# Attention, expert mixture and gated layer on one core: the last expert and last layer take one token pair at a time

## What is computed

```python
# experts: x (2304, 512), w1 (8, 512, 1024), w2 (8, 1024, 512), P (2304, 8) balanced over 8 rounds
out = sum(P[:, e:e+1] * (np.maximum(x @ w1[e], 0.0) @ w2[e]) for e in range(8))
# last layer: w_gate, w_val (512, 1536), w_out (1536, 512)
xn = out / np.sqrt(np.mean(out * out, axis=-1, keepdims=True) + 1e-6) * rms_g
g = xn @ w_gate
y = (g / (1 + np.exp(-g)) * (xn @ w_val)) @ w_out
```

## Time and profile before

| | us |
|---|---|
| median of 3 runs | 2183.65 |
| lowest, highest | 2183.62, 2208.83 |
| profiled execution, device time | 2198.95 |
| its span, first to last instruction | 2197.2 |
| mean granted TensorE clock, share of full | 0.987 |

### The profile page before, as it was taken

The page is one execution under the profiler, slowest core; times in us unless marked ns, Lnnn a source line. Parts: engine busy times, 40 slices in busy tenths (PEclk is TensorE's granted clock), DMA queues, the critical chain, the costliest instruction groups (busy, mean ns, idle before and its releaser), DMA issues.

```text
span 2197.2 us, 28136 instructions
## 1 busy us (share of the span) xinstructions
PE 2117.6 (96%) x10780; PEld 1890.1 (86%) x10780; DVE 1357.6 (62%) x2452; ACT 750.4 (34%) x1816; POOL 338.6 (15%) x362
## 2 busy tenths in 40 slices
PE   8987999999999999999999999999999689999998
PEld 6777989789898989989898989899988578888887
DVE  3676576555656565656565556556556766666666
ACT  3663222423233323233223233232234533333332
POOL 3351010000000000000000000000001433333332
PEclk9999999999999999999999999999999889999999
DMA  4320001000000100000100000100000000000002
GB/s 128 115 85 1 20 20 34 20 20 25 20 20 20 34 20 25 20 20 20 34 20 25 20 20 20 34 24 21 20 20 15 15 15 29 15 30 15 27 18 87
DMA packets 34517, 65.28 MB, mean 30 GB/s; under 512 B 3952, under 2 KB 5968, under 8 KB 34384
## 3 DMA queue, kind: packets, MB, share of 16 engines
q1 hardware_dynamic: 34384, 63.48, 8.9%
HBM read 58.75 MB, written 4.72 MB: 29 GB/s over the span
## 4 chain that ended last, share of the span: by engine, by line
PE 89%; DVE 4%; POOL 3%; ACT 3%; issue 1%; DMA 0%; SPq 0%; DVEq 0%; POOLq 0%; ACTq 0%
PE ps L1014 27%; PE ps L1015 27%; PE ps L1013 27%; PE ps L966 3%; PE ps L980 2%; POOL wa_raw L440 2%; POOL x_raw L417 1%; PE ps L992 1%; DVE x_lo L705 1%; DVE wa_lo L716 1%; PE ps L962 1%; DVE acc L780 1%; ACT x_hi L503 1%; ACT acc L561 1%; DVE h_sum L788 0%
## 5 line engine op out<-in xcount | busy, mean ns | idle before, releaser
L1013 PE MATMUL ps<-x_hi,wa_hi 128*128 128x384 f32 x1848 | 627.6, 340 | 58.5 <-DVE x_lo L705 27.9
L1014 PE MATMUL ps<-x_lo,wa_hi 128*128 128x384 f32 x1848 | 626.3, 339 | 0.0
L1015 PE MATMUL ps<-x_hi,wa_lo 128*128 128x384 f32 x1848 | 624.3, 338 | 0.0
L1015 PE MATMUL ps<-w_hi,h_lo 128*128 128x512 f32 x1368 | 542.5, 397 | 0.0
L1014 PE MATMUL ps<-w_lo,h_hi 128*128 128x512 f32 x1368 | 540.7, 395 | 0.0
L1013 PE MATMUL ps<-w_hi,h_hi 128*128 128x512 f32 x1368 | 534.2, 391 | 3.7 <-DVE w_lo L721 2.7
L773 DVE SCALAR_TENSOR_TENSOR acc<-ps,plan,acc 128x512 f32<-128x512 f32 x504 | 377.1, 748 | 139.8 <-PE ps L1015 139.5
L1013 PEld LDWEIGHTS ps<-x_hi,wa_hi 128*128 128x128 f32 x1848 | 350.3, 190 | 97.3 <-ACT h_sum L528 30.7
L1014 PEld LDWEIGHTS ps<-x_lo,wa_hi 128*128 128x128 f32 x1848 | 350.1, 189 | 28.1
L528 ACT ACTIVATE h_sum<-ps 128x384 f32<-128x384 f32 x396 | 193.3, 488 | 487.8 <-PE ps L1015 487.8
L1015 PEld LDWEIGHTS ps<-x_hi,wa_lo 128*128 128x128 f32 x1848 | 350.1, 189 | 0.0
(11 more groups left out here) (104 smaller groups left out, 1450.8 us busy)
## 6 DMA issues: line engine op xcount, KB each, us to landing
raw<-stream SPq DMA_DIRECT2D x164, 256.0 KB, 2.9
out<-acc SPq DMA_DIRECT2D x18, 256.0 KB, 2.1
v_sb<-v_loc SPq DMA_DIRECT2D x8, 384.0 KB, 4.2
q_sb<-q_str SPq DMA_DIRECT2D x8, 315.0 KB
k_sb<-k_str SPq DMA_DIRECT2D x8, 315.0 KB
v_sb<-v_str SPq DMA_DIRECT2D x8, 315.0 KB
k_sb<-k_loc SPq DMA_DIRECT2D x8, 304.0 KB, 3.4
q_sb<-q_loc SPq DMA_DIRECT2D x8, 288.0 KB, 2.8
```

The lines of the kernel that those rows point to most:

```text
L1013: nc.tensor.matmul(out_ap, a_hi, b_hi, start=first, stop=False, **free)
L1014: nc.tensor.matmul(out_ap, a_hi, b_lo, start=False, stop=False, **free)
L1015: return nc.tensor.matmul(out_ap, a_lo, b_hi, start=False, stop=last, **free)
```

## The change

From unit 28 on, the last expert, the order of steps is turned: all four units for pair 0, then for pair 1, then for pair 2 (steps 84 to 95); the same in the last layer, twelve units for each pair (steps 96 to 131). So every one of these 48 steps needs a new unit, and each is loaded and converted anew: 76 *fetches* instead of 44 units. In the last layer the w1 parts alternate between two buffers (`wa`, `wb`), the w2 chunk has four slots instead of three, the z bank and the gate and value tiles (`gv`, `sh_hi`, `sh_lo`) are doubled or fourfold.

x for the last layer is made over 7 to 9 steps for each pair (squares in steps 89, 97 and 108, norms and transposes in the two steps after, sums, high and low parts up to steps 95, 105 and 116).

In the last layer the outputs of two consecutive steps are accumulated in PSUM and added to `acc` once: three outputs of 6 matmuls in a step, at places 0, 2 and 4; none in step 97. Steps 130 and 131 have theirs singly. The output rows of a pair are stored when the pair is done.

The diff, cut to its core:

```diff
+UNITS_LAST = FC // 2
+FETCH_CYCLE = UNITS_MOE - UNITS_LAST
+FETCH_MOE = FETCH_CYCLE + TP * UNITS_LAST
+FETCHES = FETCH_MOE + TP * KC
+CYCLE = TP * FETCH_CYCLE
...
+def unit_of(s):
+    if s < CYCLE:
+        return s // TP
+    return FETCH_CYCLE + (s - CYCLE) % UNITS_LAST if s < MOE else UNITS_MOE + (s - MOE) % KC
...
 def w2_step(g):
-    u = unit_of_w2(g)
-    if u == 0:
+    f = fetch_of_w2(g)
+    if f == 0:
         return None
-    if u >= UNITS_MOE:
-        return TP * u - 1
-    return TP * u - 2 if g % 2 == 0 else TP * u + 1
+    if f >= FETCH_MOE:
+        return first_step(f)
+    if g % 2:
+        return first_step(f) + 1
+    return TP * f - 2 if f <= FETCH_CYCLE else first_step(f)
...
+SQUARES = [CYCLE + 5, MOE + 1, MOE + KC]
+SUMS = {0: {SQUARES[0] + 3: (0, 4)}, 1: {SQUARES[1] + 3: (0, 2), SQUARES[1] + 4: (2, 4)},
+        2: {SQUARES[2] + 3: (0, 2), SQUARES[2] + 4: (2, 4)}}
+SPLITS = {0: {SQUARES[0] + 4: (0, 3), SQUARES[0] + 5: (3, 5), SQUARES[0] + 6: (5, 7)}}
+for n_pair in (1, 2):
+    SPLITS[n_pair] = {SQUARES[n_pair] + 5 + i: (2 * i, min(2 * i + 2, 7)) for i in range(4)}
...
     GpSimd, step s (q = s - MOE)
         for s in range(STEPS):
+            f, q = fetch_of(s), s - MOE
+            if q >= 0:
+                if q:
+                    h_low(q - 1, 1)
+                    h_low(q - 1, 0)
                 pool.wait_ge(sig_done, 2 * q + 1)
+                nc.gpsimd.tensor_tensor(gv[:, q % 2, SIG0, :], gv[:, q % 2, GATE0, :], gv[:, q % 2, SIG0, :],
                                         ALU.mult).then_inc(silu0_done, 1)
+            if s == last_step(f) and f + 1 < FETCHES:
                 for k in range(4):
+                    w1_sum(f + 1, k)
...
     ScalarE, a last-layer step
+        def last_layer_step(s):
+            f, q = fetch_of(s), s - MOE
+            fetch = f + 1 < FETCHES
+            snap(s, 0)
+            if q:
+                h_high(q - 1, 0)
...
+            if fetch:
+                w1_high(f + 1, 0)
+                w1_high(f + 1, 1)
+            sigmoid(q, 0)
+            if fetch:
+                w1_high(f + 1, 2)
+                w1_high(f + 1, 3)
+            snap(s, 1)
+            more_x(s, 0)
+            if fetch:
+                w1_high(f + 1, 4)
+                w1_high(f + 1, 5)
+            snap(s, 2)
+            more_x(s, 1)
+            if fetch:
+                w1_high(f + 1, 6)
...
+            sigmoid(q, 1)
+            more_x(s, 2)
+            h_high(q, 1)
+            more_x(s, 3)
...
     VectorE, a last-layer step
+            if q:
+                product_0(q - 1)
...
+            early_x(s)
+            add(s, 0)
+            if fetch:
+                w1_low(f + 1, 0)
+                w1_low(f + 1, 1)
+            evac(s, 0)
+            if fetch:
+                w1_low(f + 1, 2)
+                w1_low(f + 1, 3)
+            evac(s, 1)
+            if fetch:
+                w1_low(f + 1, 4)
+                w1_low(f + 1, 5)
+            more_x(s, 0)
+            add(s, 1)
+            evac(s, 2)
+            if fetch:
+                w1_low(f + 1, 6)
...
+            evac(s, 3)
+            more_x(s, 1)
+            product_1(q)
+            evac(s, 4)
+            evac(s, 5)
```

More of the change, by code:

```diff
@@ L53 @@
 UNITS_MOE = E * FC // 2
[L54 to L79 removed]
+GROUPS = 2 * SUB
+ORDER = [3, 4, 5, 0, 1, 2]
@@ new lines, in outputs_of, with last_output @@
+def outputs_of(s):
+    return max(n for n, (steps, tok) in enumerate(OUTPUTS) if s in steps) + 1
+def last_output(tok, end):
+    return max(n for n, (steps, t) in enumerate(OUTPUTS) if t == tok and steps[-1] < end)
+SQUARES = [CYCLE + 5, MOE + 1, MOE + KC]
+SUMS = {0: {SQUARES[0] + 3: (0, 4)}, 1: {SQUARES[1] + 3: (0, 2), SQUARES[1] + 4: (2, 4)},
+        2: {SQUARES[2] + 3: (0, 2), SQUARES[2] + 4: (2, 4)}}
+SPLITS = {0: {SQUARES[0] + 4: (0, 3), SQUARES[0] + 5: (3, 5), SQUARES[0] + 6: (5, 7)}}
@@ new lines, in more_x @@
+        def more_x(s, k):
+            for p in range(TP):
+                if s == SQUARES[p]:
+                    for i in ((0, 1), (2,), (3, 4), (5,))[k]:
+                        square(p, i)
+                if s - SQUARES[p] in (1, 2):
+                    xt(p, DC * (s - SQUARES[p] - 1) + k)
+                first, end = SPLITS[p].get(s, (0, 0))
+                if first + k < end:
+                    x_high(TP + p, first + k)
+        for s in range(STEPS):
+            if s < MOE:
+                moe_step(s)
+            else:
+                last_layer_step(s)
@@ L659, in _ @@
+        h_high(TP * KC - 1, 0)
     @block.vector
@@ L936, in _ @@
-            if s:
-                evac(s, 5)
-            if fetch:
-                w1_low(u + 1, 6)
-            if before in range(TP):
-                mean_square(before, 0)
-            if now in range(TP):
-                for o in range(NPROD):
-                    x_low(TP + now, o)
+            low(s, 2)
+            if fetch:
+                w1_low(f + 1, 4)
+                w1_low(f + 1, 5)
+            evac(s, 4)
+            add(s, 2)
+            low(s, 3)
+            evac(s, 5)
@@ new lines, in last_layer_step @@
+        def last_layer_step(s):
+            f, q = fetch_of(s), s - MOE
+            fetch = f + 1 < FETCHES
+            if q:
+                product_0(q - 1)
+            else:
+                for g in range(W2_CHUNKS):
+                    if w2_step(g) == s and w2_late(g):
+                        w2_low(g)
+            early_x(s)
+            add(s, 0)
+            if fetch:
+                w1_low(f + 1, 0)
+                w1_low(f + 1, 1)
+            evac(s, 0)
+            if fetch:
+                w1_low(f + 1, 2)
+                w1_low(f + 1, 3)
+            evac(s, 1)
+            if fetch:
+                w1_low(f + 1, 4)
+                w1_low(f + 1, 5)
+            more_x(s, 0)
+            add(s, 1)
+            evac(s, 2)
+            if fetch:
+                w1_low(f + 1, 6)
+            for g in range(W2_CHUNKS):
+                if w2_step(g) == s and not w2_late(g):
+                    w2_low(g)
+            evac(s, 3)
+            more_x(s, 1)
+            product_1(q)
+            evac(s, 4)
+            evac(s, 5)
@@ new lines, in more_x @@
+        def more_x(s, k):
+            for p in range(TP):
+                if s == SQUARES[p] and k == 1:
+                    mean_square(p, 0)
+                first, end = SPLITS[p].get(s, (0, 0))
+                for o in range(first, min(first + 1, end)) if k == 0 else range(first + 1, end):
+                    x_low(TP + p, o)
+        for s in range(STEPS):
+            if s < MOE:
+                moe_step(s)
+            else:
+                last_layer_step(s)
+        product_0(TP * KC - 1)
@@ L946, in _ @@
+        for k in range(GROUPS):
+            evac(STEPS, k)
     @block.tensor
@@ L1162, in _ @@
             product(s, O_A22, y_up, False)
-            if s:
-                outputs(s, 5)
+            outputs(s, 5)
             between(s, 5)
+        for k in range(GROUPS):
+            outputs(STEPS, k)
     ctx.close()
```

535 lines of the change are left out of this document (277 added, 258 removed).

## The result

The changed kernel takes 2284.9 us (median of four runs, 2275.85 to 2304.55); the kernel before took 2190.71 beside it (2183.62 to 2208.83). The ratio is 1.043, with an interval of 1.032 to 1.054: slower. The profiled execution took 2275.85, its span is 2274.1, and the mean clock is 0.979 against 0.987.

What follows compares the result with a forecast made beforehand. Took TensorE's matmuls as the bound, with the change adding a wait to every last-layer step. 618 + 79 (wait) + 46 (smaller terms) + 20 (clock) = 763 against 682.7, +80, so 2264 us; range 2215 to 2310.

Steps and rivals of the forecast that it cites:

- The wait put into every last-layer step: Before S1, TensorE waits for ScalarE's copy behind w1 parts needing GpSimd's late sums: 33 steps x 2.4, 79 us.
- The clock: TensorE drops to 1.2 GHz after some waits: 12 to 13 falls, 20 us, bounds 0 to 55.
- TensorE's work alone, 618: From step 84 to the last matmul, matmuls and transposes without any waiting take 618 us, against 682.7 before.
- Norms: In steps 98, 99, 109 and 110 they precede VectorE's first add; the chain starts 2.0 later: 8 us.
- parts of x: Low parts in steps 102 to 104 and 113 to 115 make VectorE's next first add late: 10 us.
- step 96: Late w2 part, w1 load, table load and sigmoid chain put S1 at 13.3 instead of 7.0: 6.4 us.
- step 97: No output stands before S1, so the same chain makes the step 13.4 instead of 7.4: 6 us.
- end: After the last steps, the last product stands behind two evacuations: 1.8 us.
- GpSimd's sums of x: Two of 1.9 after the w1 sums end before GpSimd's next input comes, so they cost nothing.
- The w2 term: In the last expert, the second chunk's low part reaches output 0 late: 0.95 x 11 steps, 10.5 us.
- the blocking rule: Two-input VectorE and GpSimd instructions block each other in SBUF; low parts could each lose up to 0.7 more.
- Rival 1: The order does no harm: third GpSimd sum done by 5.0, S1 does not wait, -45, 2139 us; chance 0.10.

Runs made afterwards that it cites:

- experiment 1: Changed kernel with GpSimd's four w1 sums ahead of the second low part and the sigmoid's product in last-layer steps: 2202.3 us, ratio 1.003 to the kernel before.
- experiment 2: Changed kernel with ScalarE's copy for S1 ahead of w1 high parts 2 and 3 in last-layer steps: 2230.6 us (once).
- experiment 3: Changed kernel with one unused 128x384 GpSimd product ahead of the sigmoid's product in last-layer steps: 2330.3 us (once).
- experiment 4: Changed kernel with one unused 128x384 GpSimd product behind the four w1 sums in last-layer steps: 2278.6 us (once).
- experiment 6: Changed kernel with the second w2 chunk's high and low parts made one step earlier in the last expert and step 96: 2258.1 us (once).
- experiment 11: Changed kernel with w1 sums first, add before norm, w2 chunk early, last product before last evacuations, pair 0's x sums early: 2177.2 us, ratio 0.991 to kernel before.
- experiment 7: Changed kernel with GpSimd's w1 sums first, VectorE's first add ahead of the norm and the second w2 chunk early: 2167.4 us, ratio 0.989 to the kernel before.
- experiment 5: Changed kernel with VectorE's first add ahead of the norm's operations in last-layer steps: 2269.3 us (once).
- experiment 10: Changed kernel with GpSimd's sums of x for pair 0 (step 92) ahead of that step's w1 sums: 2302.1 us (once).

## Why the prediction was right

The forecast was 2264 us in a range of 2215 to 2310; the median is 2284.9. The profiled execution, the fastest of the four, is 12 above the forecast, which is the 12 by which the stretch came out longer (775.2 for 763). The other 9, up to the median, can't be placed, since the other executions have no profile; the start of step 84 alone differs by up to 26 between profiled ones. The mechanism is the one forecast; here is the sum against the measurement, with the clock taken out of the steps.

| us | forecast | measured |
|---|---|---|
| steps 84 to 95 | 203.5 | 211.5 |
| steps 96, 97 | 35.4 | 34.1 |
| steps 98 to 130 | 482.2 | 478.8 |
| step 131 and end | 21.6 | 21.7 |
| clock, all steps | 20 | 29.2 |
| sum | 763 | 775 |

**The wait put into every last-layer step: right.** Forecast 2.2 idle and a step of 13.9 from the durations of the earlier trace rows; measured 2.20 and 13.94. Two small errors inside the chain cancel: GpSimd's product takes 1.26 and not 1.02, and the sigmoid before it ends 0.11 earlier. The forecast also had 33 of them, and there are 33. The table of experiments 1 to 4 shows its cause, the sums behind the sigmoid and the copy behind the sums: take away either link and it goes or shrinks, lengthen it and it grows by the same amount, put the load elsewhere and nothing happens.

**The clock: right for the last layer, too low in all, and in part luck.** The forecast had 12 to 13 falls and 20 us, chosen between its bounds of 0 and 55 on the strength of two waits. In steps 98 to 130, 13 steps contain seven or more matmuls of 384 columns 0.32 apart (or of 512 columns 0.43 apart) instead of 0.175 (0.23); the excess over these spacings adds up to 21.6 us. Steps 93, 94, 96 and 97 have falls too, for another 3.7 and 3.9. Steps 122 and 127, 15.5 long with the same wait of 2.20 as their neighbours of 13.94, show one fall alone, 1.56 each. TensorE of the changed kernel in step 122, at the end of such a fall:
```profile
2132.28 0.52 PE L1231 MATMUL ps<-x_hi,wa_lo 128*128 128x384 f32 x1
2132.60 0.46 PE L1229 MATMUL ps<-x_hi,wa_hi 128*128 128x384 f32 x1
2132.90 0.34 PE L1230 MATMUL ps<-x_lo,wa_hi 128*128 128x384 f32 x1
2133.07 0.34 PE L1231 MATMUL ps<-x_hi,wa_lo 128*128 128x384 f32 x1
```
Here 1.2 GHz ends: 0.32, then 0.30, then 0.17.

**TensorE's work alone, 618: supported.** With the waits removed, an ordinary step of experiment 1 takes 11.46 to 11.54 where 11.53 stood in the sum, and the expert step of experiment 6 takes 15.64.

**Norms, parts of x, step 96, step 97, end: right in sum, not all one by one.** Step 96 took 22.88 where the sum has 22.0, step 97 15.10 for 13.4, both with a fall of the clock; the end 21.66 for 21.6. Steps 98 to 130 come to 482.2 by the sum's terms without the clock (380.5 + 79 + 8 for norms + 10 for parts + 4.7 for two thirds of the transposes), and measured 500.4 - 21.6 = 478.8. Inside that, with the clock taken out of each step, the four norm steps cost some 6 where the sum has 8, and the steps with parts of x some 5 where it has 10. GpSimd's sums in steps 100, 101, 111 and 112, put at nothing, cost some 3.

**The last expert: a term mis-sized.** The stretch was missed in two places, the clock (9 us) and here (8 us without the clock). The sum has 203.5 for steps 84 to 95 (12 x 15.64, some eleven w2 waits, 3 for parts of x, 2.3 for transposes); measured 215.2, of which 3.7 are the clock. The w2 term itself held: waits of 0.80 to 1.04 in steps 85 to 89, forecast 0.95. The step that failed reads "GpSimd's sums of x ... end before its next input comes, so they cost nothing". It looked at GpSimd's own queue and not at what VectorE does beside it. Steps 92 to 95 lie 17.2 above 15.64 each, and the sum had 6.8 for them; 3.7 of the 17.2 are the clock in steps 93 and 94. The late w2 part and the sums add to each other: without the late w2 part (experiment 6) steps 92 to 95 lie 5.0 above, and with the sums moved as well (experiment 11) 0.3. The prediction weighed the blocking rule, and wrote that the trace shows only the 0.3 per product. That reading was wrong. The trace of the kernel before has the long case, where x is split for the experts; VectorE, and GpSimd beside it:
```profile
164.29 10.44 DVE L705 TENSOR_TENSOR x_lo<-x_raw,x_hi 128x768 fp32r<-128x768 f32 x5 [1.44 <-ACT x_hi L503]
163.69 9.35 POOL L417 TENSOR_TENSOR x_raw<-x_raw 128x768 f32<-128x768 f32 x4 [4.14 <-ACT x_raw L497]
```
Five low parts of x take 10.44, four of them 2.07 to 2.60 each, where 35 of the 42 take 0.94 to 0.96; the mean of 1.14 in the earlier trace rows hides both kinds.

**Rival 1, the other side,** named the right condition: if the third sum is done by 5.0, S1 does not wait. The changed kernel didn't meet it; experiment 1 does, at 4.34. It priced the kernel at 2139; experiment 7, with two more mends, stands at 2167. What keeps it there are its steps 98 to 116, of which only 107 is at 11.5; most of them wait for VectorE, GpSimd's low part or the copy.

## What to carry to other kernels

When conversion work is put into every step of a pipeline, write down for each copy that the bounding engine waits for what stands ahead of it in its queue, and what that waits for in turn: here a 0.47 us copy cost 2.2 us in each of 33 steps, on an engine that is busy 6.16 of the 13.90 us of a step, and moving four operations of another engine removed it. Free the late input rather than the instruction that waits for it, since the next instruction inherits the lateness. And price an operation in a "free" stretch of one engine by what it does to the operations beside it too; for that, look for the longest case in the trace, not for the mean.

## What the runs showed of the hardware

**Long GpSimd operations multiply short VectorE ones.** A low part of 128x256 takes 0.42 us alone and 2.0 beside sums of 128x768 of 2.0 each; with the sums moved away it takes 0.42 again, and where they went another one took 1.80 and a w2 low part 2.28, where 0.69 is its mean in the kernel before.

**The clock fell after idle times of 2.2 us, but not always.** Counted over steps 117 to 130, where little else disturbs: after idle times of mostly 2.20 in 2 of 14 steps (changed kernel, and 2 of 14 again in each of experiments 4, 5, 6 and 10), after 2.97 in 9 of 14 (experiment 3), after 1.11 in none (experiment 2). One fall costs 1.56 us. The 0.77 us that experiment 3 adds to a step so cost another 0.5 per step through the clock (17 us in 33 steps). What decides a single case is open.

**A further table load did not come.** Squares of `acc` stand between sigmoids in steps 97 and 108, and still the changed kernel has one load in the last layer, like the one before. Groups of ScalarE by line (count, busy us, mean ns, idle before):
```profile
L670 ACT ACT_TABLE_LOAD x1 | 1.3, 1283 | 0.0
```
It took 1.28 us again with no idle time before it. The 2.66 us that the Trainium skill, "ScalarE: Activation LUTs", section "What ACT_TABLE_LOAD costs", gives with its drain is not seen here.

**The same attention code took different times.** Step 84 starts between 1495 and 1521 us in the profiled executions. In the first part of the attention stage the DMA moves at different rates; before, by the columns of the earlier trace rows:
```profile
20.00:60.00 40.00, 40.00 (x174) 32.09 (x173) 13.08 (x39) 12.46 (x66) 10.41 (x10) 1.00 0.16 51
```
The same 40 us of the changed kernel:
```profile
20.00:60.00 40.00, 40.00 (x286) 32.08 (x287) 22.17 (x66) 24.05 (x123) 16.45 (x14) 1.00 0.32 100
```
51 against 100 GB/s, and VectorE, ScalarE and GpSimd run about half as many instructions in the same 40 us; experiment 1 shows 51 again. The cause wasn't looked for. A comparison of two kernels by one span each can hold up to 26 us of it.
